# Two tiles of the first product share one pass over the array, 64 rows each

## The reference

```python
# x: (4, 4096, 192), weight_gen: (4, 4096, 8, 7), w_in: (192, 2048), w_out: (2048, 192), all float32
w = exp(weight_gen - max over the 7 taps);  w = w / (sum over taps + 1e-9)      # softmax, 8 heads, 7 taps
out[b, s, head h] = sum over k of w[b, s, h, k] * x_padded[b, s + k, head h]    # 6 zero rows ahead of x, 24 channels a head
x = out.reshape(16384, 192)
h = x @ w_in                                  # first product, 192 -> 2048
g = h * clip(h + 3, 0, 6) / 6                 # the gate
return g @ w_out                              # second product, 2048 -> 192
```

## Time and profile before

| | |
|---|---|
| runs | 3, median 1226.82 us (1226.55 to 1227.56) |
| the profiled execution, first to last instruction (span) | 1224.4 us |
| a median run less that span | 2.4 us |
| busy share PE, PEld, DVE, ACT, POOL | 98%, 88%, 66%, 52%, 56% |
| granted TensorE clock, mean of the span | 0.999 |

### The profile page before, as it was taken

How to read it: one execution, slowest core, us unless ns; L and a number is a source line. 1 busy time by engine, 2 the same in 40 slices (tenths; PEclk the granted TensorE clock), 3 DMA queues, 4 the chain that set the end, 5 groups by cost and what they waited for, 6 DMA issues and landing times.

```text
span 1224.4 us, 19650 instructions
## 1 busy us (share of the span) xinstructions
PE 1194.6 (98%) x6848; PEld 1083.3 (88%) x6848; DVE 803.7 (66%) x1362; ACT 634.2 (52%) x1269; POOL 690.8 (56%) x455
## 2 busy tenths in 40 slices
PE   1999999999999999999999999999999999999998
PEld 1899999999999999999999999999999999998997
DVE  7866657576665766656666575766657666566665
ACT  3455555455555555545555554555555555455554
POOL 7893854909358192762918549094581927729100
PEclk9999999999999999999999999999999999999999
DMA  6101010010101001010010100101010010100000
GB/s 179 46 22 58 20 45 13 20 58 20 58 0 65 14 20 58 0 65 13 20 58 20 45 13 20 58 20 58 0 56 22 20 58 0 65 13 13 13 14 13
DMA packets 12071, 42.08 MB, mean 34 GB/s; under 512 B 1183, under 2 KB 5279, under 8 KB 10139
## 3 DMA queue, kind: packets, MB, share of 16 engines
q1 hardware_dynamic: 12059, 41.93, 9.8%
HBM read 29.34 MB, written 12.58 MB: 34 GB/s over the span
## 4 chain that ended last, share of the span: by engine, by line
PE 96%; DVE 1%; POOL 1%; issue 0%; DMA 0%; ACT 0%; DVEq 0%; ACTq 0%
PE work L464 48%; PE sums L482 32%; PE sums L484 15%; PE work L444 2%; POOL pool_acc L154 0%; POOL pool_prod L152 0%; DVE w_in L404 0%; DMA w_raw<-weight_gen_dram 0%; DVE work L350 0%; DVE w_out L410 0%; DVE g_lo L361 0%; DVE out_stage L381 0%; POOL pool_acc L147 0%; POOL pool_prod L148 0%; DVE xt_b L373 0%
## 5 line engine op out<-in xcount | busy, mean ns | idle before, releaser
L350 DVE SCALAR_TENSOR_TENSOR work<-relu,work 128x512 f32<-128x512 f32 x512 | 355.2, 694 | 402.9 <-ACT relu L254 402.8
L482 PE MATMUL sums<-w_out,g_hi 128*128 128x384 f32 x2048 | 614.1, 356 | 0.7 <-DVE g_lo L361 0.7
L254 ACT ACTIVATE relu<-work 128x512 f32<-128x512 f32 x512 | 306.4, 598 | 554.0 <-PE work L464 549.3
L484 PE MATMUL sums<-w_out,g_lo 128*128 128x192 f32 x2048 | 513.0, 251 | 0.0
L464 PE MATMUL work<-xt_a,w_in 128*128 128x512 f32 x1536 | 449.3, 400 | 2.0 <-DVE xt_b L373 2.0
L482 PEld LDWEIGHTS sums<-w_out,g_hi 128*128 128x128 f32 x2048 | 384.3, 188 | 23.7 <-DVE g_lo L361 1.3
L484 PEld LDWEIGHTS sums<-w_out,g_lo 128*128 128x128 f32 x2048 | 389.8, 190 | 15.8
L361 DVE TENSOR_TENSOR g_lo<-work,g_hi 128x512 fp32r<-128x512 f32 x512 | 349.7, 683 | 2.1
L464 PE MATMUL work<-xt_b,w_in 128*128 128x512 f32 x1024 | 318.1, 392 | 0.0
L264 ACT CAST g_hi<-work 128x512 fp32r<-128x512 f32 x512 | 299.3, 585 | 11.4 <-DVE work L350 11.3
L147 POOL TENSOR_TENSOR pool_acc<-x_in,w_soft 128x768 f32<-128x768 f32 (+1 forms) x32 | 50.0, 1563 | 442.7 <-DVE w_soft L341 429.7
(11 more groups left out here) (31 smaller groups left out, 203.7 us busy)
## 6 DMA issues: line engine op xcount, KB each, us to landing
x_in<-x_dram SPq DMA_DIRECT2D x15, 1344.0 KB, 6.0
out_dram<-out_stage SPq DMA_DIRECT2D x32, 384.0 KB, 2.8
w_raw<-weight_gen_dram SPq DMA_DIRECT2D x16, 224.0 KB, 3.0
w_out_raw<-moe_w_out_dram SPq DMA_DIRECT2D x1, 1152.0 KB, 13.5
x_in<-x_dram SPq DMA_DIRECT2D x1, 768.0 KB, 5.1
w_in_raw<-moe_w_in_dram SPq DMA_DIRECT2D x1, 768.0 KB, 8.9
w_in_raw<-moe_w_in_dram SPq DMA_DIRECT2D x2, 384.0 KB, 10.3
w_out_raw<-moe_w_out_dram SPq DMA_DIRECT2D x1, 384.0 KB, 6.6
```

Of the source, the lines that this page charges most:

```text
L254: nc.scalar.activation(t.relu[:, m % 2, :], t.work[m % BANKS][:], ACT.Relu, bias=3.0).then_inc(s.relu_ready, 1)
L350: nc.vector.scalar_tensor_tensor(bank[:], t.relu[:, m % 2, :], 6.0, bank[:], ALU.min, ALU.mult).then_inc(s.gated, 1)
L482: nc.tensor.matmul(t.sums[n][:, 0:2 * D], t.g_hi[:, m % BANKS, cols], t.w_out[:, j, :], start=(j == 0), stop=False)
L484: ins = nc.tensor.matmul(t.sums[n][:, D:2 * D], t.g_lo[:, m % BANKS, cols], t.w_out[:, j, 0:D], start=False, stop=(j == TILES - 1))
```

## The change

`attend` now writes `attn_b` with each token's 64 channels twice in a row (128 columns a group instead of 64), so that each of four 128x128 transposes gives the same 64 rows in partitions 0 to 63 and again in 64 to 127. ACT writes the high part of the upper copy to `xt_b` rows 0 to 63 and of the lower copy to a new tensor `xt_c`, rows 64 to 127; DVE writes the low part to `xt_b` rows 64 to 127. The fourth pass of a tile is as before. In place of the fifth, the fill of an even slot m starts with two matmuls over 64 rows of the array each, which read w_lo against x_hi: rows 0 to 63 for slot m and rows 64 to 127 for slot m + 1, into the two slots' banks. They open both banks, so the fill of slot m now waits until the bank of slot m + 1 is free too (`bank_free`).

```diff
@@ attend
-    for out, c0, c1 in ((t.attn_a, 0, DA), (t.attn_b, DA, D)):
-        eng.tensor_tensor(by_token(out[:, half, t0 * (c1 - c0):t1 * (c1 - c0)], c1 - c0), ...
-                          ALU.add).then_inc(ready, 1)
+    eng.tensor_tensor(by_token(t.attn_a[:, half, t0 * DA:t1 * DA], DA), *last_terms(0, DA), ALU.add).then_inc(ready, 1)
+    twice = t.attn_b[:, half, t0 * P:t1 * P].rearrange("p (n o c) -> p n o c", o=2, c=DB)
+    eng.tensor_tensor(twice, *[a.unsqueeze(2).broadcast_to([P, t1 - t0, 2, DB]) for a in last_terms(DA, D)],
+                      ALU.add).then_inc(ready, 1)
@@ scalar_program, x_hi
-            for odd in range(2):
-                nc.scalar.copy(block_b(t, half, odd, odd), pairs_of(bank, odd)).then_inc(s.xt_hi_ready, 1)
+            for out, rows in ((t.xt_b, slice(0, DB)), (t.xt_c, slice(DB, P))):
+                nc.scalar.copy(out[rows, half, :], bank[rows, :]).then_inc(s.xt_hi_ready, 1)
@@ vector_program, x_lo
-            for odd in range(2):
-                nc.vector.tensor_tensor(block_b(t, half, odd, 1 - odd), pairs_of(bank, odd),
-                                        f32(block_b(t, half, odd, odd)), ALU.subtract).then_inc(s.xt_lo_ready, 1)
+            for cols in (slice(0, N // 2), slice(N // 2, N)):
+                nc.vector.tensor_tensor(t.xt_b[DB:P, half, cols], bank[DB:P, cols],
+                                        f32(t.xt_c[DB:P, half, cols]), ALU.subtract).then_inc(s.xt_lo_ready, 1)
@@ tensor_program, transpose_set
-        for i in range(GT if what == TA else GT // 2):
+        for i in range(GT):
@@ tensor_program, fill
-                    (t.w_in[:, 1, 0, cols], t.xt_a[:, half, 0, :]), (t.w_in[:, 0, 1, cols], t.xt_b[:, half, :]),
-                    (t.w_in[:, 1, 1, cols], t.xt_b[:, half, :])]
+                    (t.w_in[:, 1, 0, cols], t.xt_a[:, half, 0, :]), (t.w_in[:, 0, 1, cols], t.xt_b[:, half, :])]
+        second = m % 2 == 1
+        if not second:
+            if m >= AHEAD:
+                bank_free(q, m - AHEAD, last)
+            for rows, x, i in ((slice(0, DB), t.xt_b, m), (slice(DB, P), t.xt_c, m + 1)):
+                j = slot(i)[1]
+                nc.tensor.matmul(t.work[i % BANKS][:], t.w_in[rows, 1, 1, j * P:(j + 1) * P], x[rows, half, :],
+                                 start=True, stop=False)
         for i, (w, x) in enumerate(products):
-            ins = nc.tensor.matmul(bank[:], w, x, start=(i == 0), stop=(i == len(products) - 1))
+            ins = nc.tensor.matmul(bank[:], w, x, start=False, stop=(i == len(products) - 1))
         ins.then_inc(s.filled, 1)
+    def bank_free(q, m, last):
+        if skipped(m, last):
+            return
+        if is_tile(m):
+            pe.wait_ge(s.g_lo_ready, tiles_done(q, m))
+        else:
+            pe.wait_ge(s.xt_lo_ready, inputs_split(q, m))
```

More of the change, by code:

```diff
@@ L112, in by_tap @@
     return ap.rearrange("p (n k) -> p n k", k=K)
[L115 to L125, removed]
 def across_taps(ap):
@@ L155, in attend, with last_terms @@
     eng.wait_ge(step, steps + ATTN_STEPS)
-    for out, c0, c1 in ((t.attn_a, 0, DA), (t.attn_b, DA, D)):
-        eng.tensor_tensor(by_token(out[:, half, t0 * (c1 - c0):t1 * (c1 - c0)], c1 - c0),
-                          by_token(accs[:, half, t0 * D:t1 * D], D)[:, :, c0:c1],
-                          by_token(prods[:, (K - 1) % 3, t0 * D:t1 * D], D)[:, :, c0:c1],
-                          ALU.add).then_inc(ready, 1)
+    def last_terms(c0, c1):
+        return (by_token(accs[:, half, t0 * D:t1 * D], D)[:, :, c0:c1],
+                by_token(prods[:, (K - 1) % 3, t0 * D:t1 * D], D)[:, :, c0:c1])
+    eng.tensor_tensor(by_token(t.attn_a[:, half, t0 * DA:t1 * DA], DA), *last_terms(0, DA), ALU.add).then_inc(ready, 1)
+    twice = t.attn_b[:, half, t0 * P:t1 * P].rearrange("p (n o c) -> p n o c", o=2, c=DB)
+    eng.tensor_tensor(twice, *[a.unsqueeze(2).broadcast_to([P, t1 - t0, 2, DB]) for a in last_terms(DA, D)],
+                      ALU.add).then_inc(ready, 1)
 def sync_program(nc, sp, dram, t, s):
@@ L568, in __init__ @@
         self.attn_a = sb("attn_a", [P, 2, GT * DA])
-        self.attn_b = sb("attn_b", [P, 2, GT * DB])
+        self.attn_b = sb("attn_b", [P, 2, GT * P])
         self.ident = sb("ident", [P, P])
@@ L572, in __init__ @@
         self.xt_b = sb("xt_b", [P, 2, N], F32R)
+        self.xt_c = sb("xt_c", [P, 2, N], F32R)
         self.w_in_raw = sb("w_in_raw", [P, 2, FF])
```

## The result

The changed kernel takes 1299.27 us (median of 4, 1299.02 to 1299.71) against 1226.68 us: ratio 1.0592, 95% interval [1.0577, 1.0607], so 72.6 us slower. The forecast was 14 us slower; the direction was right, the size was not, and the time lies just inside the upper end of the stated range (1207 to 1300 us). The profiled execution has a span of 1297.2 us, 72.8 above the one before.

A forecast was written before the change was run, and what follows sets the result against it. TensorE, 98% busy, was taken as the bound. Pair -30.2, transposes +7.0, moved wait +26.4, smaller waits +10, start +1 gave +14.2 us on 1224.4; with 2.4 us beside the span, 1241.0 us, range 1207 to 1300.

The forecast's parts named there:

- The pair: Two 64-row matmuls replacing two fifth passes (0.468 us): taken at 0.350 us, 256 times, 30.2 us saved.
- The bound from above: Dearest pair: each of two shape switches waits for work in flight, then loads openly; 0.766 us, 76.3 us lost.
- the drained case: Rival: TensorE drains at both switches around a pair, 1348 us, or at one, 1282 us; chance 0.17 together.
- two signs of being wrong: Forecast wrong if the 0.85 us TensorE gap ahead of slot 16's pair is missing, or a pair costs under 0.295 us.
- the serial rival: The pair's two matmuls run one after the other, saving nothing: 1271 us, chance 0.10.
- the single switch: Only one of a pair's two shape switches drains: 0.510 us a pair, 1282 us; most of a 0.17 chance.
- the second bound: Pair's matmuls stream together but the second weight load is uncovered: 0.324 us a pair, 36.9 us saved.
- Rival 1: Not slower: pair's matmuls start within 0.02 us, both loads covered, 54.8 us saved; 1216 or 1191 us, chance 0.28.
- The moved wait: Slot 16's fill, now opening slot 17's bank, waits for DVE's low part of TB: 0.85 us each, +26.4 us.
- The smaller waits: Pairs at slots 18 and 22 wait for DVE's low parts of slots 15 and 19: +10 us taken, 16 at most.
- The transposes: Two more TensorE transposes in each of 32 sets TB, 0.22 us a set: +7.0 us.
- What is hidden: POOL's last addition writes 512 columns, up to 0.74 us more a half, covered by POOL's waits; 23 us if uncovered.

The follow-up runs named there:

- run 1: Changed kernel with the pair's two matmuls over all 128 rows, at the same place and with the same wait: 1270.30 us, ratio 1.0357.
- run 3: Changed kernel with one 64-row matmul at the front of each tile's own fill, in place of pairs: 1427.48 us, ratio 1.1646.
- run 6: Changed kernel with the pair's two matmuls over 128 columns instead of 512, their result written over by the full passes: 1254.12 us, ratio 1.0226.
- run 2: Changed kernel with each pair issued twice in a row, the second writing over the first: 1354.31 us, ratio 1.1044.
- run 5: Kernel before the change, with four transposes in each set TB instead of two: 1233.56 us against 1226.49, ratio 1.0059.
- run 8: As run 7, but with six buffers instead of four for g_hi and g_lo: 1205.71 us against 1226.46 for the kernel before, ratio 0.9835.
- run 7: Rewrite with both products in the 64-row shape throughout, only transposes in full shape, against the kernel before: 1235.37 us, ratio 1.0071.

## Why the prediction was wrong

- **The pair, the step that failed.** "I take 0.350, between the second and the third" was 30.2 us saved; it is 0.62 us a pair and 39.3 us lost. That one term is 69.5 us off; the others together were 11 too high. The nearest row, 0.05 us behind the transposes, was read as a change of mode and was none, since a transpose there has the same 128-row shape (`128*128` in the rows) as the passes around it. The bound from above had the right parts, an array that stops and then loads in the open, twice: it put 0.256 a switch, and 0.19 was measured (0.09 standing, 0.10 loading). Run 1 shows the 0.10 of the open load by itself (the prediction's 0.09 for it was read from loads that begin under the matmul ahead, so it came close by chance); runs 3 and 6 show the whole as fixed and tied to the change. Why the next matmul starts 0.09 us late, no run shows: the tail of 0.166 that the prediction put for it is longer. What the prediction called the drained case, with 0.17 of chance, is what happened, at three quarters of its price a switch (39.3 us lost for 76.3).
- **The signs.** Neither of the prediction's two signs of being wrong came (the gap was there, and the pair didn't cost less than 0.295), for it had none for a dearer pair but "over 0.5 with a drain"; the 0.43 from the pair to the next full pass shows only half the price, since 0.09 lies ahead of the pair and 0.10 behind the full pass.
- **What was luck.** The direction rests on the terms around the pair, which measured 33.5 us for the 44.4 taken and make the kernel slower by themselves; that the pair lost time too, instead of saving it, was no part of the forecast and happened to point the same way. And the range holds 1299 only because it was drawn over the serial rival and the single switch; the full drain was left outside, though a cost at both switches is what happened; at 0.19 a switch instead of 0.256 it stays just inside.
- **That the two run together** was right, and better than assumed: 0.003 us apart, both loads at once. The second load never lies open as in the second bound. Run 2 shows the pair as one pass of 0.215. The Trainium skill's 4 ns between tiles (TensorE: Matmul & The Clock Gate, Part 3, The mechanism) agrees with the trace; the loads pulled ahead, which the same section has, are there in run 2's second pair and not in a pair that follows another shape. Rival 1 still fell, because it priced the pair by that alone and put nothing for the change of shape. The Trainium skill's rule on the other side (TensorEngine Tiling (Array Packing), Tiling Modes, Key Properties: a change of mode drains TensorE) is the one that decided. The runs agree that the change costs and add its price, 0.19 us; whether the 0.09 of it is a drain they don't show.
- **The moved wait**: right in place, cause and count. Taken 0.85 us, measured 0.66 (2.07 to 2.73), 17 to 18 us for 26.4, within the bounds 11.5 to 28.5. DVE ended at 2.67 for 2.77: the casts ended later than taken (1.87 for 1.79), DVE's two pieces took 0.77 for 0.87. The pair followed after 0.06 instead of 0.12. Of the 20.7 us of the step into slot 16, 3 are counted with the pairs as their way in; run 1 has the same step without it, so by itself the wait is worth all 20.7.
- **The smaller waits** at slots 18 and 22: taken 10 us, measured about 1 (the way in has 0.188 us in the mean and 0.182 in the median). They are there, but inside the stop. Run 1, without it, shows 6 us of them on the way in and 5 us more in the open loads behind them (62 x 0.085), 11 in all: the size was right for full rows, and what failed is that they add to the cost of the pair.
- **The transposes**: 7.0 taken, 7.1 in the trace and in run 5.
- **What is hidden** stayed hidden: POOL's last addition grew from 738 to 1294 ns and nobody waited.
- The serial rival fell with the trace (3 ns apart) and with run 2.

## What to carry to other kernels

Count the changes of the array's shape, not only the columns: here each cost about 0.19 us, so a lone pair of 512-column half-height matmuls (0.23 us saved, 0.38 lost) loses. Row tiles paid in the one kernel that stayed in them; there a half-height pass cost half a pass. And when the trace lacks the operation, a row of another mechanism is no midpoint between the bounds: keep both bounds, and give more of the chance to the one whose parts can each be named.

## What the runs showed of the hardware

- Two 64-row matmuls on different rows start 3 ns apart, with loads 3 to 10 ns apart, and take 0.215 to 0.23 us together for 512 columns (changed kernel, run 2). Matmuls of 192 columns pair as well (run 8): from one pair to the next 0.088 us (0.084 and 0.004 within the pair), as for one in full rows (0.087).
- A change of shape between 128 and 64 rows costs TensorE some 0.09 us by which the next matmul starts late and some 0.10 of open load, in either direction (run 2), with 128 columns or 512 in the pair (run 6). In runs 7 and 8 it comes with the transposes, now the odd shape: 0.18 us on the way in for 0.09 and 0.20 on the way out for 0.03.
- Within a shape a weight load can start with the matmul ahead of its own (205.69 for a matmul at 205.78); across a change it starts with its own (309.69). A load held by a wait lies open in the same way: 0.34 us to the next pass for 0.23 (run 1).
- A stop of TensorE hides waits for semaphores that fall into it: the way in to the pair showed 6 us of them once the stop was gone (run 1).
